# Turning the attention result in another bank and another slot, in a fused attention and two-MLP kernel

## The reference, cut to what matters

```python
for t in range(S):                                   # attention, per batch and head
    m_new = np.maximum(f[t] + m, i[t])
    f_stab, i_stab = np.exp(f[t] + m - m_new), np.exp(i[t] - m_new)
    C = f_stab * C + i_stab * outer(v[t], k[t]);  n = f_stab * n + i_stab * k[t];  m = m_new
    y[t] = sigmoid(o[t]) * (C @ q[t]) / np.maximum(np.abs(n @ q[t]), 1.0)
x = y as (3072, 320)
h = x @ w_in;   x = np.maximum(0.01 * h, h) @ w_out
h = x @ w2_in;  out = (h * np.cos(h)) @ w2_out
```

## Time and profile before

| what | value |
|---|---|
| three runs | 893.58, 895.42, 895.97 us; median 895.42 |
| the profiled execution | span 896.2 us; no other time of it is given, and its span is 0.2 us above the slowest of the three runs |
| busy: TensorE matmuls, weight loads | 855.6 us (95%), 837.1 us (93%) |
| busy: VectorE, ScalarE, GpSimd | 664.3 us (74%), 465.5 us (52%), 292.6 us (33%) |
| blocks 1 to 6 of the first MLP | some 62 to 64 us each |
| blocks of the second MLP | 43.6 us each, TensorE busy throughout |
| mean granted TensorE clock | 0.990 of full speed |

### The profile page before, as it was taken

How to read it: one execution, slowest core, us unless ns; L and a number is a source line. 1 busy time by engine, 2 the same in 40 slices (tenths; PEclk the granted TensorE clock), 3 DMA queues, 4 the chain that set the end, 5 groups by cost and what they waited for, 6 DMA issues and landing times.

```text
span 896.2 us, 16521 instructions
## 1 busy us (share of the span) xinstructions
PE 855.6 (95%) x5750; PEld 837.1 (93%) x5750; DVE 664.3 (74%) x1155; ACT 465.5 (52%) x1013; POOL 292.6 (33%) x288
## 2 busy tenths in 40 slices
PE   7898898999989999899999999999999999999997
PEld 6888898999989999898999998999999999999997
DVE  7698857667668577588566447888888888888885
ACT  2343343343343343433433668777767777777775
POOL 1564513221312313123010465333333333333333
PEclk9899999999999999999999999999999999999999
DMA  7376322413414323223402151111010101010000
GB/s 255 106 259 202 104 82 82 172 36 129 160 36 143 110 82 126 83 82 126 146 1 89 54 178 52 67 44 45 24 45 22 44 22 44 22 44 22 0 23 23
DMA packets 31291, 75.78 MB, mean 85 GB/s; under 512 B 3136, under 2 KB 16832, under 8 KB 31232
## 3 DMA queue, kind: packets, MB, share of 16 engines
q1 hardware_dynamic: 31232, 74.95, 24.4%
HBM read 62.95 MB, written 11.99 MB: 84 GB/s over the span
## 4 chain that ended last, share of the span: by engine, by line
PE 49%; issue 24%; POOL 13%; DVE 11%; ACT 2%; DMA 1%; SPq 0%; POOLq 0%; DVEq 0%; ACTq 0%
PE h L497 18%; POOL g_lo L1018 12%; PE acc L507 6%; PE acc L509 6%; PE acc L508 6%; PE x L474 4%; DVE nrm L780 3%; PE s L446 2%; DVE x L790 2%; PE s L457 2%; PE x L471 1%; PE s L481 1%; DVE x L786 1%; DVE x L792 1%; PE x L481 1%
## 5 line engine op out<-in xcount | busy, mean ns | idle before, releaser
L497 PE MATMUL h<-xT,w_in 128*128 128x384 f32 x1536 | 302.1, 338 | 2.7 <-issue 2.2
L497 PEld LDWEIGHTS h<-xT,w_in 128*128 128x128 f32 x1536 | 268.5, 188 | 3.6 <-issue 2.9
L507 PE MATMUL acc<-w_out,g_hi 128*128 128x320 f32 x768 | 243.6, 317 | 4.3 <-POOL g_lo L1018 4.3
L584 ACT ACTIVATE t_f<-h 128x384 f32<-128x384 f32 x192 | 94.4, 492 | 278.5 <-PE h L497 278.5
L509 PE MATMUL acc<-w_out,g_lo 128*128 128x320 f32 x768 | 237.5, 309 | 0.0
L508 PE MATMUL acc<-w_out,g_hi 128*128 128x320 f32 x768 | 236.2, 308 | 0.0
L1018 POOL TENSOR_TENSOR g_lo<-g_f,g_hi 128x384 fp32r<-128x384 f32 x128 | 131.8, 1030 | 213.1 <-ACT g_hi L584 213.1
L836 DVE TENSOR_TENSOR g_f<-h,t_f 128x384 f32<-128x384 f32 x128 | 71.0, 554 | 128.4 <-ACT t_f L584 128.3
L507 PEld LDWEIGHTS acc<-w_out,g_hi 128*128 128x128 f32 x768 | 144.5, 188 | 6.7 <-POOL g_lo L1018 3.1
L508 PEld LDWEIGHTS acc<-w_out,g_hi 128*128 128x128 f32 x768 | 144.6, 188 | 0.0
L509 PEld LDWEIGHTS acc<-w_out,g_lo 128*128 128x128 f32 x768 | 144.3, 188 | 0.0
(11 more groups left out here) (105 smaller groups left out, 907.4 us busy)
## 6 DMA issues: line engine op xcount, KB each, us to landing
qk_s<-qk SPq DMA_DIRECT2D x24, 512.0 KB, 3.4
D<-g_dram SPq DMA_DIRECT2D x24, 512.0 KB, 5.5
kvo_s<-kvo SPq DMA_DIRECT2D x24, 484.0 KB, 4.2
x_dram<-stage SPq DMA_DIRECT2D x8, 960.0 KB, 4.4
xT<-x_dram SPq DMA_DIRECT2D x8, 960.0 KB, 4.7
eG_b<-e_dram SPq DMA_DIRECT2D x48, 128.0 KB, 5.9
out<-x SPq DMA_DIRECT2D x24, 160.0 KB, 1.8
raw_in<-w1i SPq DMA_DIRECT2D x8, 384.0 KB, 5.1
```

Of the source, the lines that this page charges most:

```text
L497: last = nc.tensor.matmul(bank[:, 0:BLOCK], w(a), x[:, k, :], start=(n == 0), stop=(n == 7))
L507: nc.tensor.matmul(acc[t][:, 0:DM], g_hi[:, s, r], w_out[:, 0, j, :], start=(j == 0), stop=False)
L584: copy = lambda o, i, **k: nc.scalar.activation(o, i, ACT.Copy, **k)
```

## The change

`TURN` moves to slots 7, 10, 14 and writes bank `x` (`turn_bank`), except for block 0's own units. `SCORES` go to slots 3, 6, 10, `PROBS` to 4, 7, 11, `OUTPUTS` to 5, 8, 12, and the first MLP's result is turned in slots 4, 11, 15. A slot may now hold two unit steps; on every engine TURN comes first. Scores no longer wait for `xT_done` but for `C_done`; outputs wait for `xT_done` of the unit before in place of `x1_done`; the second and third turn of the first MLP's result wait for `xT_done` too. The store in block 7 goes behind the last weight loads.

```diff
-SCORES, PROBS, OUTPUTS, TURN, UNIT_SLOTS = 0, 1, 2, 3, 4
-UNIT_START = 3
-TURN2 = (4, 7, 11)
+UNIT_SLOTS = {SCORES: (3, 6, 10), PROBS: (4, 7, 11), OUTPUTS: (5, 8, 12), TURN: (7, 10, 14)}
+TURN2 = (4, 11, 15)
...
             for k in range(RAW_OUT, PIECES):
                 load_raw_in(w2i, PIECES + k)
-                if k == PIECES - 2:
-                    store_x2(BLOCKS - 2)
                 load_raw_out(w2o, PIECES + k)
+            store_x2(BLOCKS - 2)
             sp.wait_ge(h_done, BLOCKS * FT)
...
+        def turn_bank(b, c):
+            return score_banks(b, c)[1] if first(b, c) else x_bank
...
             def unit_scores(b, c):
                 if not first(b, c):
-                    pe.wait_ge(xT_done, unit(b, c))
+                    pe.wait_ge(C_done, b * (CHUNKS - 1) + c)
...
             def unit_outputs(b, c):
                 if not first(b, c):
-                    pe.wait_ge(x1_done, unit(b, c))
-                    pe.wait_ge(x2_split, unit(b, c) - 2)
+                    pe.wait_ge(xT_done, unit(b, c))
+                    pe.wait_ge(x2_split, unit(b, c) - 2 - (c % TILES > 0))
...
             def unit_transpose(b, c):
                 pe.wait_ge(x1_done, unit(b, c) + 1)
-                transposes(score_banks(b, c)[1], x1[:, c % 2, :], T_done)
+                transposes(turn_bank(b, c), x1[:, c % 2, :], T_done)
...
             def slot(row, i):      # TensorE; ScalarE and VectorE take the same order
...
+                if u := row.unit(i, TURN):
+                    unit_transpose(*u)
+                if u := row.unit(i, SCORES):
+                    unit_scores(*u)
+                if u := row.unit(i, OUTPUTS):
+                    unit_outputs(*u)
                 t = row.turn2(i)
                 if t is not None:
+                    if t and row.unit(i - i % FT + UNIT_SLOTS[TURN][0], TURN):
+                        pe.wait_ge(xT_done, row.block(i) * TILES + TILES + t + 1)
                     block_transpose(row.block(i) - 1, t)
```

More of the change, by code:

```diff
@@ L42 @@
 BUFS = 3
-SCORES, PROBS, OUTPUTS, TURN, UNIT_SLOTS = 0, 1, 2, 3, 4
-UNIT_START = 3
-TURN2 = (4, 7, 11)
+SCORES, PROBS, OUTPUTS, TURN = "scores", "probs", "outputs", "turn"
+UNIT_SLOTS = {SCORES: (3, 6, 10), PROBS: (4, 7, 11), OUTPUTS: (5, 8, 12), TURN: (7, 10, 14)}
+TURN2 = (4, 11, 15)
 PIECES = 8
@@ L227, in in_mlp2, with unit @@
                 return self.second_mlp or (isinstance(self.first, int) and self.tile(i) >= BLOCKS * FT)
-            def unit_step(self, i):
+            def unit(self, i, step):
                 if self.in_mlp2(i) or (isinstance(self.first, int) and self.block(i) == BLOCKS - 1):
                     return None
-                at = i % FT - UNIT_START
-                if not 0 <= at < UNIT_SLOTS * TILES:
-                    return None
-                c = (1 - self.half(i)) * TILES + at // UNIT_SLOTS
-                return self.batch + (i // FT + self.odd + 1) // 2, c, at // UNIT_SLOTS, at % UNIT_SLOTS
+                if i % FT not in UNIT_SLOTS[step]:
+                    return None
+                c = (1 - self.half(i)) * TILES + UNIT_SLOTS[step].index(i % FT)
+                return self.batch + (i // FT + self.odd + 1) // 2, c
             def starts(self, n, i):
@@ L607, in x_hi @@
                 act.wait_ge(T_done, unit(b, c) + 1)
-                round_turned(dst, score_banks(b, c)[1], c % TILES).then_inc(xh_done, 1)
+                round_turned(dst, turn_bank(b, c), c % TILES).then_inc(xh_done, 1)
             def g_round(row, i):
@@ L671, in slot @@
                         copy(x2[:, t, 0:DM], acc[t][:, 0:DM]).then_inc(acc_read, 1)
[L672 to L681, removed]
+                if u := row.unit(i, TURN):
+                    x_hi(*u, xT[:, 1 - row.half(i)])
+                if u := row.unit(i, SCORES):
+                    sigmoid_exp(*u)
+                    decays(*u)
+                if u := row.unit(i, OUTPUTS):
+                    normaliser(*u)
                 t = row.turn2(i)
@@ L823, in x_lo @@
                 dve.wait_ge(xh_done, unit(b, c) + 1)
-                split_turned(dst, score_banks(b, c)[1], c % TILES).then_inc(xT_done, 1)
+                split_turned(dst, turn_bank(b, c), c % TILES).then_inc(xT_done, 1)
             def g_rest(row, i):
@@ L830, in slot @@
             def slot(row, i):
-                step = row.unit_step(i)
-                if step and step[3] == PROBS:
-                    probs(*step[:2])
+                if u := row.unit(i, PROBS):
+                    probs(*u)
                 if exists(row, i) and not row.in_mlp2(i):
@@ L853, in slot @@
                        ALU.mult).then_inc(prod_done, 1)
[L854 to L862, removed]
+                if u := row.unit(i, TURN):
+                    x_lo(*u, xT[:, 1 - row.half(i)])
+                if u := row.unit(i, SCORES):
+                    sigmoid(*u)
+                if u := row.unit(i, OUTPUTS):
+                    state(*u)
+                    outputs(*u)
                 t = row.turn2(i)
```

## The result

The changed kernel takes 902.65 us (median of 11 runs, 897.3 to 912.91), the kernel before 895.63 us on the same chip (11 runs, 892.45 to 898.43). The ratio is 1.0075, with a 95% interval of 1.0052 to 1.0098: slower, where 877.6 us was forecast. It also scatters more: 15.6 us between its runs, against 6.0 before. Runs over 1.5% above a kernel's fastest, which show a lower mean clock (here two of eleven, 912.31 and 912.91 us at 0.967 and 0.968), are left out of every ratio, so a ratio is not quite the quotient of the medians. The profiled execution has a span of 898.3 us, and it took 900.06 us, so around a span lie some 1.8 us. It is a short one for this kernel, while the one before (896.2 + 1.8 = 898.0 us) was a long one: the two profiles differ by 2.1 us, the medians by 7.0.

A forecast was written before the change was run, and what follows sets the result against it. TensorE, busy 855.6 of 896.2 us, was taken to bound the kernel. A gross gain of 24.1 us less 6.3 us of new costs left 17.8 us: 895.4 - 17.8 = 877.6 us, range 872 to 889.

The forecast's parts named there:

- What is removed: TensorE's waits before unit turns for VectorE's last scaling go, 22.6 us, plus 1.5 us of clock: 24.1 us gross gain.
- Lengths of new slots: TensorE's slots: 4.0 us with scores, 3.04 with a turn alone, 4.3 with both, 5.4 or 6.3 with OUTPUTS.
- Outputs behind the first turn: Slot 8, outputs after the first unit turn in bank `x`: no wait, 0.6 us to spare, except in block 0.
- Slots 11 and 15: Turns of the first MLP's result there need the previous slot's split, ready 1.7 us early in slot 11: nothing lost.
- The third load behind the store: SyncE's third-unit load follows the first MLP result's store; GpSimd's L929 may delay slot 5: 0 to 0.9 us, 1.0 in all.
- Outputs behind x2's second turn: Slot 12, one slot after the first MLP result's second turn: TensorE waits for VectorE's split, 2.5 us in all.
- rival A: GpSimd's whole L929 holds VectorE's `g_lo` in slots 3 and 10, delaying slots 5 and 12: 889.7 us, chance 0.13.
- Block 0: New TensorE waits there, 0.9 us for scores and 1.3 us for outputs: 2.2 us.
- the dip that was to go: Block 0: granted clock of 0.74, then 0.61, after TensorE's 2.56 us wait; 1.5 us to be taken back.
- B: Bank `x` becomes the chain: 30 handoffs in six blocks idle 1 us each, slower, 901 us; chance 0.05.
- C: Wait only renamed: slot 6's scores wait for a `C_done` as late as `x1_done`, nothing won, 895 us; chance 0.04.
- The forecast's own signs of being wrong: New waits summing to over 12 us, or the first MLP's blocks shrinking by less than 1 us each.

The follow-up runs named there:

- the load first: Changed kernel with SyncE's load of each third unit back in slot 14, ahead of the store of the first MLP's result: 889.94 us, ratio 0.9896.
- the load held: Changed kernel with SyncE holding each third unit's load until the first product of the next block's slot 3 is done: 892.59 us, ratio 0.988.
- the wait filled: Changed kernel, third load ahead of the store, eight unused identity matmuls before slot 12's wait for bank `x`: 895.81 us, ratio 0.9998.
- the second product ahead: Changed kernel, third load held behind the loop edge, TensorE's second product before the third unit's outputs in slot 12: 880.07 us, ratio 0.9802.

## Why the prediction was wrong

**Right.** *What is removed.* No turn of units 3 to 23 waits for the scaling; slots 6 and 7 take 4.00 and 3.04 us as worked out. *Lengths of new slots*: 3.04, 6.28 and 4.35 us were measured for the forecast 3.04, 6.3 and 4.3. *Outputs behind the first turn*: slot 8 takes 6.28 us in blocks 1 to 6, no wait. *Slots 11 and 15*: no wait.

**Wrong, the step that decided: "The third load behind the store".** It was priced at 1.0 us, and cost 11.4 + 4.0 = 15.4 us: 14.4 of the 20 us by which the span was missed. The step placed SyncE's transfers rightly (split done, 0.6 us, then the load), and followed them to GpSimd's L929, to slot 5 and no further. It never asked what else uses the DMA engines at that time, and so put the effect on TensorE's loop jump at nothing, without a reason. The row for it stood in the document: the earlier trace rows has 1.03 us of idle time marked as issue before slot 3, where TensorE's loop jumps back, and the prediction took the 4.10 us of that slot as a fixed length. The runs show what it is: moving only the load onto the edge makes the kernel before slower by 1.0% (idle times 2.8 and 3.2 us), moving it off the edge in the changed kernel leaves 0.9 us idle, and with TensorE's loop written out there is no idle time at all. The code behind the jump is fetched after it, by a packet that goes through the DMA engines: it starts 1.0 to 1.6 us after the jump with no data traffic and 1.9 to 5.2 us after it with data taking 80 to 100% of them. That it stands behind the data in the engines' queues is inferred from these times. The Trainium skill's "Runtime: NRT & Kernel Launch" ("Instruction fetch mechanics") says that a taken branch whose target is not among the pages at hand breaks the sequential prefetch and waits for a DMA of the target's page. The traces agree: 0.6 to 1.2 us idle with quiet DMA engines, 1.6 to 5.0 with busy ones. Of the 11.4 us at the edges, 5.6 are this idle time, and the rest goes with the half clock behind it.
The smaller half of the step was named with its right bound: in block 2 L924 ran from 180.86, VectorE's L760 took 2.02 instead of 0.32 us, and slot 5 waited 0.43 us. The bound was 0.9, and slot 5 lost 0.8 us in blocks 4 and 6, but 2.3 in block 2, where the clock was at 0.57 over the 4 us from 190.

**Wrong in size: "Outputs behind x2's second turn".** Forecast 2.5 us, measured 7.7. Most of the miss is in the waits themselves: TensorE waits 0, 1.04, 0.71, 1.04, 1.10 and 0.50 us in blocks 1 to 6, 4.4 us in all, where 0.9 us or less was forecast in each of blocks 2 and 4, 0.4 in block 6 and 0.1 in the others, and a slot lost 0.2 to 0.5 us more than its rows say. The hold is of the kind that rival A named, but by another instruction, GpSimd's mask on VectorE's sigmoid (0.66 to 1.28 us instead of 0.32 in blocks 2 to 5), and part of it fell on the probs (L771), for which no wait was forecast. The rest, some 1.7 us, is the clock behind the wait in block 5, slot 12:

```profile
416.00:418.00 2.00, 1.98 (x18) 1.98 (x18) 1.95 (x5) 0.00 (x0) 0.43 (x1) 1.00 0.11 33
418.00:420.00 2.00, 2.00 (x14) 2.00 (x14) 0.92 (x4) 0.18 (x1) 1.86 (x2) 0.76 0.03 8
420.00:422.00 2.00, 2.00 (x9) 2.00 (x9) 1.49 (x3) 0.00 (x0) 2.00 (x4) 0.50 0.00 0
```

The forecast took the clock as something to win back in block 0 and priced every new wait at its own length. Before the change, waits of 1.1 to 1.5 us stood behind a first product and cost no clock: it was 1.00 in every window from 120 us on. The new ones of 0.4 to 1.5 us stand inside the stretch of small matmuls. Half clock followed two of the eight in slots 5 and 12 of the changed kernel, two of six with the load first, and four of five with the load held, for 3 to 7 us each. Their length does not tell which: of three waits of 0.43 us in slot 5 one was followed by it, of two of 1.04 us in slot 12 none. The kernel with the wait filled and two of the kernels with next to no wait show a clock of 1.00 in all six windows; the third, with the second product ahead, has the one dip told above. So that a wait brings the dips on is likely and not shown; what else it takes is open.

**Block 0.** 2.2 us forecast, 4.6 measured, again by the clock: 0.64 and 0.51 in windows of 4 us each from 80 us, behind a wait of 0.47 us in slot 8. So the dip that was to go only moved. This row is the least sure of the table: between the nine kernels with the moved turns slot 5 takes 6.3 to 12.4 us and slot 8 7.3 to 13.1, their sum 15.7 to 19.7, though some of these share their code there.

**Rivals.** B's sign came true, but not its mechanism: no chain over bank `x` formed. A's mechanism did in slot 5, and with another instruction in slot 12, without its size. C did not. The forecast's own signs of being wrong came: the new waits and what hung on them sum to over 12 us, and blocks 2, 4, 5 and 6, from slot 3 to slot 3, grew by 1.1 to 4.3 us where each was to shrink by 2 to 3 (blocks 1 and 3 did shrink, by 4.0 and 1.5). The mechanism that made it slower was on no list.

**The forecast itself.** With the load held off the edge and next to no wait in slot 12, the same moved turns of the units give 879 to 880 us, ratio 0.9812 and 0.9802, near the 877.6 forecast (0.980). These are other schedules than the one that was forecast, so the nearness bears out the gain and not the sum. The gain was there, 24.7 us in the slots; side effects ate it. That the prediction took a span for a time (its profiled run took 898.0 us, not 896.2) changes nothing, since it went by the difference.

## What to carry to other kernels

When a change moves when a transfer is issued, follow the transfer's own interval, not only its consumers: look for a loop's jump of the bounding engine under it, and keep large loads some microseconds off it, or write the loop out. Price a new wait by where it stands, and not by its own length alone: a wait of 1.20 us before a turn cost 1.36 us here, one of 0.43 us among the small matmuls of slot 5 cost 0.8, and 2.3 where half clock followed. Moving the waiting work, or putting useful work ahead of it, took these waits away in two kernels; filling one with matmuls of no use left its slot 1.8 us or more over need.

## What the runs showed of the hardware

- TensorE's loop jump left the engine idle for 0.6 to 1.2 us with quiet DMA engines and for 1.6 to 5.0 us with busy ones. The packet of code that it waits for started 1.0 to 1.6 and 1.9 to 5.2 us after the jump. Behind idle times of 3.2 to 5.0 us the clock was lower (8 matmuls took 2.65 to 2.92 us instead of 1.7).
- TensorE's granted clock went to half behind some waits of 0.4 to 1.5 us that stood in slots 5 and 12, among their matmuls of 41 to 128 columns, and stayed full behind all waits of 1.1 to 1.5 us that stood after a first product, before a turn. Once it went to half there with no wait at all.
- Between 50 and 890 us the clock was at half for 27 us in the changed kernel's profile, in five stretches, and for 3 us in one stretch before. The runs scatter with it: 892 to 898 us before, 897 to 913 after, with a mean clock of 0.980 in the shortest and 0.964 in the one of 910.75 us.
